# Expert routing with fused VectorE steps, slots rounded to tiles in floating point, and the second layer's input loaded partly in halves

## What is computed

```python
def _moe_ref(x, w_skip, w_gate, w1, w2):
    do_compute = x @ w_skip > 0
    xc = x[do_compute]
    logits = xc @ w_gate
    e_idx = np.argmax(logits, axis=1)
    probs = softmax(logits); gate_w = probs[arange, e_idx]
    y[e_idx == e] = gate_w * (np.maximum(xc @ w1[e], 0.0) @ w2[e])
    out[do_compute] = xc + y            # other rows: out = x

def _moe2_ref(x, w_gate, w_output_gate, w1, w2):
    # the same without the skip and without adding x;
    # y is scaled by gate_w * sigmoid(x @ w_output_gate)[e] as well
```

## Time and profile before

| | |
|---|---|
| median of 3 runs | 690.13 us (688.09 to 690.76) |
| profiled execution | 688.13 us, its span 686.4 us |
| TensorE matmul busy | 658.4 us (96%) |
| TensorE weight load busy | 564.5 us (82%) |
| VectorE busy | 409.9 us (60%) |
| ScalarE busy | 337.0 us (49%) |
| GpSimd busy | 295.2 us (43%) |
| routing of layer 1, first logits step to first w1 matmul | 268.6 to 297.9 us |
| routing of layer 2, load of x issued to first w1 matmul | 434.7 to 469.5 us |

### The profile page before, as it was taken

The page is one execution under the profiler, slowest core; times in us unless marked ns, Lnnn a source line. Parts: engine busy times, 40 slices in busy tenths (PEclk is TensorE's granted clock), DMA queues, the critical chain, the costliest instruction groups (busy, mean ns, idle before and its releaser), DMA issues.

```text
span 686.4 us, 15791 instructions
## 1 busy us (share of the span) xinstructions
PE 658.4 (96%) x5939; PEld 564.5 (82%) x5949; DVE 409.9 (60%) x859; ACT 337.0 (49%) x507; POOL 295.2 (43%) x287
## 2 busy tenths in 40 slices
PE   8989999999999989899999999989999999999995
PEld 5569889888888876479998998547999999999894
DVE  7878888788888857755454635375245254443421
ACT  4568999999999886331334312232213213231200
POOL 4357999989999871021221322002132132122121
PEclk9999999999999999999999999999999999999999
DMA  9301231111220439748489964654545654941000
GB/s 279 94 2 47 55 86 49 47 48 48 60 82 25 143 129 334 280 131 310 160 301 349 349 241 142 233 208 130 192 160 173 248 174 172 372 176 51 19 31 32
DMA packets 45988, 105.77 MB, mean 154 GB/s; under 512 B 5459, under 2 KB 11603, under 8 KB 45936
## 3 DMA queue, kind: packets, MB, share of 16 engines
q1 hardware_dynamic: 38464, 87.65, 36.8%
q0 software_dynamic: 4544, 12.70, 5.8%
q10 hardware_dynamic: 2928, 4.72, 2.0%
HBM read 87.64 MB, written 13.11 MB: 147 GB/s over the span
## 4 chain that ended last, share of the span: by engine, by line
PE 53%; DVE 3%; DMA 2%; issue 1%; ACT 0%; POOL 0%; POOLq 0%; ACTq 0%; DVEq 0%
PE hT_ps_layer L1381 27%; PE y_ps_layer L1394 7%; PE y_ps_layer L1398 7%; PE y_ps_layer L1401 7%; PE x_turn_layer L1368 2%; DMA x<-x_mid 1%; PE hT_ps_layer L1310 1%; PE hT_ps_layer L1308 1%; PE x_turn_layer L1298 1%; DVE row_one_hot_layer L1210 1%; DMA x_tile_layer<-x_src,token_to_read_layer 1%; PE hT_ps_layer L1323 1%; DMA x_mid<-y_out_layer,y_token_layer 0%; PE count_ps_layer L1298 0%; PE rank_ps_layer L1298 0%
## 5 line engine op out<-in xcount | busy, mean ns | idle before, releaser
L1381 PEld LDWEIGHTS hT_ps_layer<-xT_layer,w 128*128 128x128 f32 x1664 | 189.6, 192 | 3.8 <-DVE xT_layer L1243 1.7
L1381 PE MATMUL hT_ps_layer<-xT_layer,w 128*128 128x128 f32 x1664 | 190.2, 275 | 0.8 <-issue 0.8
L438 POOL TENSOR_TENSOR probs_lo<-probs,probs_hi 128x768 f16<-128x768 f32 x89 | 146.1, 1649 | 33.0 <-ACT probs_hi L353 30.4
L1132 ACT ACTIVATE hT_hi_layer<-hT_ps_layer 128x512 fp32r<-128x512 f32 x52 | 31.1, 597 | 239.2 <-PE hT_ps_layer L1381 239.2
L565 DVE TENSOR_REDUCE max_halves<-turn 128x1 f32<-128x384 f32 x180 | 94.7, 553 | 31.8 <-PE turn L729 30.2
L1270 DVE SCALAR_TENSOR_TENSOR hT_lo_layer<-hT_ps_layer,hT_hi_layer 128x512 fp32r<-128x512 f32 x52 | 34.6, 689 | 88.0 <-ACT hT_hi_layer L1132 77.0
L345 ACT ACTIVATE probs<-scores 128x768 f32<-128x768 f32 x96 | 79.9, 832 | 11.3 <-PE scores L753 10.3
L1445 POOL DMA_INDIRECT out_dram<-y_out_layer,y_token_layer x16 | 19.7, 1234 | 147.1 <-DVE y_out_layer L1281 147.1
L353 ACT ACTIVATE probs_hi<-scores 128x768 f16<-128x768 f32 x96 | 80.2, 836 | 1.2 <-PE pv L777 0.9
L1127 ACT ACTIVATE w_hi<-w 128x1024 fp32r<-128x1024 f32 x64 | 62.4, 1047 | 26.6 <-issue 26.6
L1250 DVE TENSOR_TENSOR w_lo<-w,w_hi 128x1024 fp32r<-128x1024 f32 x64 | 74.0, 1219 | 0.0
(11 more groups left out here) (227 smaller groups left out, 1087.5 us busy)
## 6 DMA issues: line engine op xcount, KB each, us to landing
w<-in_moe_w_dram SPq DMA_DIRECT2D x32, 2048.0 KB, 11.2
w<-in_v_dram ACTq DMA_DIRECT2D x4, 768.0 KB, 7.1
qk_raw<-in_q_dram SPq DMA_DIRECT2D x16, 192.0 KB, 3.2
qk_raw<-in_k_dram SPq DMA_DIRECT2D x16, 192.0 KB, 3.5
qB<-qA SPq DMA_DIRECT2D x16, 192.0 KB, 2.7
kB<-kA SPq DMA_DIRECT2D x16, 192.0 KB, 3.1
x_src<-x SPq DMA_DIRECT2D x2, 1536.0 KB, 17.0
x_mid<-x SPq DMA_DIRECT2D x2, 1536.0 KB, 18.3
```

The costliest lines, as they stand in the source:

```text
L438: nc.gpsimd.tensor_tensor(p_lo[slot][:], probs[slot][:], p_hi[slot][:], ALU.subtract).then_inc(p_lo_pool, 1)
L1381: t = nc.tensor.matmul(hp[n][:, i * P:(i + 1) * P], W1[par][:, c, f * P:(f + 1) * P], xT[:, c, :], start=(c == 0), stop=(c == CD - 1))
```

## The change

- The comparison with the maximum is made on `z` (is it 0), in one instruction with the product by the order numbers; the skip is one instruction with the conversion to bf16; the f32 one-hot is gone, the bf16 one is used in its place.
- A slot's tile is found without integers: a large constant, 3 x 128 x 2^22, is added, whose floating-point neighbours are 128 apart, so that the sum is rounded to tiles. The row in the tile comes out negated (`st[:, 2, :]`), and the column numbers run from 0 down to -127, now in bf16.
- The skipped tokens' offset is a ninth column of `slots`, summed with the others.
- The row one-hots are twelve instructions of 128 columns, each with a per-partition scalar, in place of two of 768 columns; TensorE waits for each. They stand ahead of the tile table, which stood ahead of them.
- The sums of the gate (of the exponentials in both layers, of the selected output gate in layer 2) are moved behind the token numbers.
- The first third of x in layer 2 is loaded in two halves of 256 columns on each queue, the second with a semaphore of its own.

```diff
--- before.py
+++ after.py
@@ -18,6 +18,8 @@
 N_EXPERTS = 8
 NO_TILE = 1 << 10
 NO_TOKEN = 1 << 11
+
+TO_TILES = P * 3 << 22
 N_TOKENS = 1536
 
 RING = 4
@@ -956,7 +958,6 @@
 
     TURNS = 4
     NG, GT = NM // 4, 4
-    HM = NM // 2
     wgs = sb("gate_weights_hi_lo", [P, CD, 2 * G], F32R)
     xh = [sb(f"xT_hi{i}", [P, GT * P], F32R) for i in range(TURNS)]
     xl = [sb(f"xT_lo{i}", [P, GT * P], F32R) for i in range(TURNS)]
@@ -964,11 +965,12 @@
     lgs = sb("gate_logits", [P, NM, G], F32)
     eq = sb("gate_best", [P, NM, E], F32)
     eqw = sb("gate_best_first", [P, NM, E], F32)
-    one_hot = sb("expert_one_hot", [P, NM, E], F32)
+    best = sb("expert_best", [P, NM, E], F32)
+
+    slots = sb("expert_slots", [P, NM, E + 1], F32)
     one_hot_b = sb("expert_one_hot_b", [P, NM, E], BF16)
     z = sb("gate_shifted", [P, NM, E], F32)
     st = sb("route_stats", [P, 12, NM], F32)
-    rank_i = sb("rank_in_expert", [P, 3, NM], I32)
     count = sb("expert_count", [P, 4, E], F32)
     over = sb("over", [P, E, thr.shape[1]], F32)
     before = sb("tiles_before", [P, E, E], F32)
@@ -1079,10 +1081,14 @@
         for par in range(2):
             expert(E // 2 - 1, par)
 
+    X_PARTS = (2, 1, 1)
+
     def x_group(dma, b, g):
 
         src = x_copy.rearrange("(b p t) d -> b p t d", b=Xt.shape[2], p=P)[b][:, 2 * g:2 * g + 2, :]
-        dma.dma_start(Xt[:, 2 * g:2 * g + 2, b, :], src).then_inc(x_loaded[g], 16)
+        for i in range(X_PARTS[g]):
+            d = slice(i * DM // X_PARTS[g], (i + 1) * DM // X_PARTS[g])
+            dma.dma_start(Xt[:, 2 * g:2 * g + 2, b, d], src[:, :, d]).then_inc(x_loaded[g if i == 0 else NG], 16)
 
     with nc.Block() as blk:
         @blk.sync
@@ -1156,27 +1162,21 @@
             gate = lgs[:, :, gate_at:gate_at + E]
             link(nc.vector.tensor_reduce(st[:, 0, :], gate, AX.X, ALU.max))
             nc.vector.tensor_tensor(z[:], gate, bc(st[:, 0, :]), ALU.subtract).then_inc(shifted, 1)
-            link(nc.vector.tensor_tensor(one_hot[:], gate, bc(st[:, 0, :]), ALU.is_equal))
-
-            link(nc.vector.tensor_tensor(eqw[:], one_hot[:], tie[:, 0:E].unsqueeze(1).to_broadcast([P, NM, E]), ALU.mult))
+            dve.wait_ge(shifted, 1)
+            link(nc.vector.scalar_tensor_tensor(out=eqw[:], in0=z[:], scalar=0.0, in1=tie[:, 0:E].unsqueeze(1).to_broadcast([P, NM, E]),
+                                                op0=ALU.is_equal, op1=ALU.mult))
             link(nc.vector.tensor_reduce(st[:, 1, :], eqw[:], AX.X, ALU.max))
-            link(nc.vector.tensor_tensor(one_hot[:], eqw[:], bc(st[:, 1, :]), ALU.is_equal))
             if first:
-                link(nc.vector.tensor_scalar(st[:, 2, :], lgs[:, :, 0:1].rearrange("p m o -> p (m o)"), 0.0, None, ALU.is_gt))
-                link(nc.vector.tensor_tensor(one_hot[:], one_hot[:], bc(st[:, 2, :]), ALU.mult))
-            nc.vector.tensor_copy(one_hot_b[:], one_hot[:]).then_inc(mask_done, 1)
+                link(nc.vector.tensor_tensor(best[:], eqw[:], bc(st[:, 1, :]), ALU.is_equal))
+                nc.vector.scalar_tensor_tensor(out=one_hot_b[:], in0=lgs[:, :, 0:1].to_broadcast([P, NM, E]), scalar=0.0, in1=best[:],
+                                               op0=ALU.is_gt, op1=ALU.mult).then_inc(mask_done, 1)
+            else:
+                nc.vector.tensor_tensor(one_hot_b[:], eqw[:], bc(st[:, 1, :]), ALU.is_equal).then_inc(mask_done, 1)
 
 
             if first:
 
-                link(nc.vector.tensor_scalar(st[:, 11, :], st[:, 2, :], -float(P * NO_TILE), float(P * NO_TILE), ALU.mult, ALU.add))
-            else:
-                link(nc.vector.tensor_tensor(eqw[:], one_hot[:], lgs[:, :, E:2 * E], ALU.mult))
-                link(nc.vector.tensor_reduce(st[:, 5, :], eqw[:], AX.X, ALU.add))
-                dve.sem_inc(sel_done, 1)
-            dve.wait_ge(exp_done, 1)
-            link(nc.vector.tensor_reduce(st[:, 3, :], eq[:], AX.X, ALU.add))
-            link(nc.vector.tensor_scalar_add(st[:, 4, :], st[:, 3, :], 1e-9))
+                link(nc.vector.tensor_scalar(slots[:, :, E:E + 1], lgs[:, :, 0:1], 0.0, float(P * NO_TILE), ALU.is_le, ALU.mult))
 
 
             K = thr.shape[1]
@@ -1192,29 +1192,36 @@
             dve.wait_ge(ranked, 1)
             link(nc.vector.scalar_tensor_tensor(out=eqw[:], in0=count[:, 3, :].unsqueeze(1).to_broadcast([P, NM, E]), scalar=float(P),
                                                 in1=rank_ps, op0=ALU.mult, op1=ALU.add))
-            link(nc.vector.tensor_tensor(eqw[:], eqw[:], one_hot[:], ALU.mult))
-            link(nc.vector.tensor_reduce(st[:, 9, :], eqw[:], AX.X, ALU.add))
-            if first:
-                link(nc.vector.tensor_tensor(st[:, 9, :], st[:, 9, :], st[:, 11, :], ALU.add))
-            link(nc.vector.tensor_copy(rank_i[:, 0, :], st[:, 9, :]))
-            link(nc.vector.tensor_scalar(rank_i[:, 2, :], rank_i[:, 0, :], 7, None, ALU.logical_shift_right))
-            nc.vector.tensor_scalar(rank_i[:, 1, :], rank_i[:, 0, :], P - 1, None, ALU.bitwise_and).then_inc(row_known, 1)
+            some = slice(0, E + 1 if first else E)
+            link(nc.vector.tensor_tensor(slots[:, :, 0:E], eqw[:], one_hot_b[:], ALU.mult))
+            link(nc.vector.tensor_reduce(st[:, 9, :], slots[:, :, some], AX.X, ALU.add))
+
+            link(nc.vector.tensor_scalar(st[:, 11, :], st[:, 9, :], 0.5 - P / 2, float(TO_TILES), ALU.add, ALU.add))
+            nc.vector.scalar_tensor_tensor(out=st[:, 2, :], in0=st[:, 11, :], scalar=float(TO_TILES), in1=st[:, 9, :],
+                                           op0=ALU.subtract, op1=ALU.subtract).then_inc(row_known, 1)
             wide = lambda a: a.unsqueeze(2).to_broadcast([P, NM, NT_COLS])
-            link(nc.vector.tensor_tensor(tile_hot[:], wide(rank_i[:, 2, :]), tile_no[:].unsqueeze(1).to_broadcast([P, NM, NT_COLS]), ALU.is_equal))
+            link(nc.vector.tensor_tensor(tile_hot[:], wide(st[:, 11, :]), tile_no[:].unsqueeze(1).to_broadcast([P, NM, NT_COLS]), ALU.is_equal))
             nc.vector.tensor_tensor(tile_tok[:], tile_hot[:], wide(tok_no[:]), ALU.mult).then_inc(toks_hot, 1)
+
+            dve.wait_ge(row_known, 1)
+            for m in range(NM):
+                nc.vector.tensor_scalar(row_hot[:, m, :], cols[:], st[:, 2, m:m + 1], None, ALU.is_equal).then_inc(rows_hot, 1)
             link(nc.vector.tensor_scalar_add(count[:, 2, :], count[:, 1, :], 1.0))
             link(nc.vector.tensor_copy(table[:], count[:, 2:4, :]))
             dve.sem_inc(table_done, 1)
-            dve.wait_ge(row_known, 1)
-            for m in range(0, NM, HM):
-                nc.vector.tensor_tensor(row_hot[:, m:m + HM, :], rank_i[:, 1, m:m + HM].unsqueeze(2).to_broadcast([P, HM, P]),
-                                        cols[:].unsqueeze(1).to_broadcast([P, HM, P]), ALU.is_equal).then_inc(rows_hot, 1)
 
 
             dve.wait_ge(toks_turned, 1)
             nc.vector.tensor_scalar(read_tok[:], tok_ps, float(NO_TOKEN), float(n_tok - 1), ALU.add, ALU.min).then_inc(to_read, 1)
             nc.vector.tensor_scalar(send_tok[:], tok_ps, float(NO_TOKEN), None, ALU.add).then_inc(to_send, 1)
 
+            if not first:
+                link(nc.vector.tensor_tensor(eqw[:], one_hot_b[:], lgs[:, :, E:2 * E], ALU.mult))
+                link(nc.vector.tensor_reduce(st[:, 5, :], eqw[:], AX.X, ALU.add))
+                dve.sem_inc(sel_done, 1)
+            dve.wait_ge(exp_done, 1)
+            link(nc.vector.tensor_reduce(st[:, 3, :], eq[:], AX.X, ALU.add))
+            link(nc.vector.tensor_scalar_add(st[:, 4, :], st[:, 3, :], 1e-9))
             if first:
                 link(nc.vector.reciprocal(st[:, 8, :], st[:, 4, :]))
             else:
@@ -1290,8 +1297,8 @@
         def _(pe):
             def route_turn(k):
                 g, c = divmod(k, CD)
-                if not first and c == 0:
-                    pe.wait_ge(x_loaded[g], 32)
+                if not first and c * X_PARTS[g] % CD == 0:
+                    pe.wait_ge(x_loaded[g if c == 0 else NG], 32)
                 if k >= TURNS:
                     pe.wait_ge(r_lo, k - TURNS + 1)
                 for i in range(GT):
@@ -1348,8 +1355,7 @@
 
             pe.wait_ge(toks_hot, 1)
             for m in range(NM):
-                if m % HM == 0:
-                    pe.wait_ge(rows_hot, m // HM + 1)
+                pe.wait_ge(rows_hot, m + 1)
                 t = nc.tensor.matmul(tok_ps, row_hot[:, m, :], tile_tok[:, m, :], start=(m == 0), stop=(m == NM - 1))
             t.then_inc(toks_turned, 1)
             warm(8)
@@ -1480,10 +1486,10 @@
         tie_b = sb("tie_b", [P, C], BF16)
         thr = sb("thresholds", [P, K_THR], F32)
         below = sb("experts_before", [P, E, E], F32)
-        cols = sb("column_number", [P, P], F32)
+        cols = sb("column_number_below_zero", [P, P], BF16)
         tri = sb("partitions_above", [P, P], BF16)
         ones_b = sb("ones_b", [P, P], BF16)
-        tile_no = sb("tile_number", [P, NT_COLS], F32)
```

(7 more changed lines are left out.)

## The result

Over 22 executions each, the kernel after took 691.97 us (median) and the one before 690.47: a ratio of 1.0033 with an interval of 1.0019 to 1.0047. The prediction had 689.0 against 690.13, a ratio of 0.998. So it was wrong: a gain of 1.1 us was forecast, and a loss was measured, of 1.5 us by the medians and of 2.3 by the ratio. The miss is 2.6 to 3.4 us. The profiled execution took 692.57 us (before: 688.13), with a span of 690.8 and a granted clock of 0.989 (before: 0.998).

What follows compares the result with a forecast made beforehand. The prediction took TensorE's gapless expert tiles as untouched, so only the two routing stages between them could change. Layer 1 -1.18, layer 2 -0.20, halves +0.30 gave -1.1 us: 689.0 against a median of 690.13, range 686.3 to 691.0.

Steps and rivals of the forecast that it cites:

- a wait or an allocation moves work elsewhere: Rival: the change is not what it seems, or over 3.4 us comes from the tile loops; either way, 5%.
- A, from the logits to the counts: Routing, z to the first step on the counts: shorter by 0.70 us in layer 1, 0.96 in layer 2.
- B, from the ranks to the one-hots: Routing, line 1193 to the first row one-hot: shorter by 0.93 us in layer 1, 0.72 in layer 2.
- C and D, the one-hots and what follows: Twelve row one-hots take 2.24 us, not 1.84, losing 0.40 a layer; from there to the token numbers costs 0.02.
- rivals at 0.106 and at 0.27 apart: Row one-hots: at 0.106 us each, 687.2 us in all (20%); at 0.27 each, 691.1 us (10%).
- The token numbers: VectorE's token numbers in routing start 1.21 us earlier in layer 1 and 1.26 in layer 2.
- E, the moved sums: Gate sums behind token numbers: 0.49 us in layer 1, nearly covered; 1.06 in layer 2, all paid, first tile gains 0.20.
- F, the halves: Layer 2's load of x, first third in halves: second group lands later, costing 0.3 us, bounds 0 and 0.5.
- the first group's arrival is worth nothing: Layer 2's load of x: TensorE waits again for the second group, so only that one's arrival counts.
- gate path isn't what layer 2 waits for: Rival, layer 2 routing: fillers shrink or the gather rules, so the moved 1.06 us is hidden; 688.0 us, 10%.
- halves gain 0.3: Rival, layer 2's load of x: first steps start earlier, second group no later; 0.3 us gained, 688.4 us, 12%.
- slow one-hots: Rival: row one-hots run at the two-tensor rate plus the scalar, 3.3 us a layer; 691.1 us, 10%.

Runs made afterwards that it cites:

- after + 32 bytes: Kernel after with 32 unused bytes a partition ahead of hT_hi in layer 2, no instruction changed: 690.14 us, 0.9989 of the kernel before.
- after + fillers: Kernel after with 14 blank matmuls instead of 8 behind the token numbers, layer 2 only: 690.2 us, 0.9998 of the kernel before.
- before + gap: Kernel before with 2 blank matmuls instead of 8 behind the token numbers in layer 2: 692.14 us, 1.0034 of the kernel before.
- 32 bytes ahead of x: Kernel after with 32 unused bytes a partition ahead of x, moving everything behind it: 691.76 us in one execution.

## Why the prediction was wrong

- **What bounds the kernel.** The tile loops were taken as a row of TensorE work that the change can't touch. It touched them by where its tensors lie: +1.5 us in layer 2 (after + 32 bytes takes it back), about -0.4 in layer 1. The rival "a wait or an allocation moves work elsewhere" named it at 5%, without a price.
- **A, from the logits to the counts.** Right: -0.63 (forecast -0.70) and -0.97 (-0.96). The 0.07 in layer 1 is a slip of the sum: the mask at 283.41 instead of 284.05 is 0.64, and the counting behind it didn't change.
- **B, from the ranks to the one-hots.** Right: -0.92 (-0.93) and -0.71 (-0.72). Prices of dependent steps, read from rows 4 and 5, carried over to the new ones here within 0.01 us in all.
- **C and D, the one-hots and what follows.** Right in kind; the term was mis-sized. The twelve start 0.163 us apart and are 248 ns long, 2.04 us where 2.24 were forecast, and the stretch to the token numbers grew by 0.24 and 0.25 instead of 0.42. The rivals at 0.106 and at 0.27 apart both fall. By the Trainium skill's rate for bf16 ("VectorE: DVE Perf Modes", section "The perf-mode tier table") the prediction's estimate was 0.17, and that was the nearer one.
- **The token numbers.** 1.31 and 1.44 us earlier, forecast 1.21 and 1.26.
- **E, the moved sums.** Layer 1 right: -1.34 in all against -1.18. In layer 2 the delay was right: token numbers to first transposes grew by 1.19 us (after + fillers, 5.83 against 4.64), forecast 1.06. (Some 0.4 of it came back between the transposes and the first w1 matmul, which is 7.34 us behind the token numbers instead of 6.55.) The step that failed stands one sentence on: "All of the 1.06 is paid: the token numbers gain 1.26, the first tile gains 0.20." It took an idle TensorE for a mere delay. Its wait ahead of the gate matmuls became 2.59 us long, and behind it fillers and transposes ran at 1.2 GHz: 1.2 + 0.5 = 1.7 us more, shown by before + gap and by after + fillers. At the full clock the first tile does gain, 0.64 us; with the clock lost it is 1.03 later. The prediction had the idle time in its rows and let the clock be, because the profiled execution had 1.00 in both routing stages.
- **F, the halves.** Right in sign, short in size: 0.5 to 0.65 us of load where 0.30 was forecast, and 0.99 in the profiled pair. The prediction priced the packets and kept the further issue for its upper bound of 0.5; the second group was in fact issued 0.54 us later, and its load took 0.11 longer, where 0.3 was put on the packets. The step that failed besides is "the first group's arrival is worth nothing": it is worth less than nothing, since an early start only makes the wait behind it longer, and behind that wait the clock fell in four profiles of eight, 1.6 us each time.
- **The median and the profile.** The 2.0 us between them were carried along as they were. They are the clock that most executions lose, mostly in attention: 0.994 against 0.998 is 2.8 us of 690. The prediction could have asked what this one execution lacked.
- **The sum.** Of the 2.6 to 3.4 us missed, the clock at layer 2's gate is 1.7, in full, since a fall there cost the kernel before nothing; the tiles are 1.5 - 0.4 = 1.1; the halves' load 0.2 to 0.35 beyond the forecast, and the clock behind them 4/8 x 1.6 = 0.8; the routing steps were better than thought by 0.16 and 0.44. That makes 3.2 to 3.4 us, and the interval of the ratio is 1.0 us either way. The shares of executions that lose the clock come from few profiles each and are the weak part of this sum: in attention, without fillers there, it fell in 6 of 9 profiles built on the kernel after and in 2 of 4 built on the one before.

The rival that the gate path isn't what layer 2 waits for fell: the chain still goes over the gate parts. The rival that the halves gain 0.3 fell as well. That of slow one-hots had a time near the measured one (691.1), by luck: its mechanism didn't happen.

## What to carry to other kernels

Where a step is moved, check what the engine behind it does while it waits: a longer idle TensorE doesn't only cost its length, it can cost the clock of what follows, and a few blank matmuls over the wait give that back. Don't read a clock of 1.00 in one execution as a property of the kernel; set the profiled execution's time against the median and ask what the difference is made of. Any edit that adds or resizes a buffer can move hot operands against one another, so compare the period of an untouched loop before and after, and if it differs try a pad before blaming an instruction.

## What the runs showed of the hardware

- The granted clock fell to 0.50 (1.2 GHz) for 3.4 us (6.8 in before + gap) at idle times of TensorE of 2.5 to 2.6 us ahead of the gate matmuls, in seven profiles of seven, and in four of eight behind 1.7 to 3.2 us at the load of x in halves. With 1.3 us or less ahead of the gate and added fillers it held in six of six. No length of the wait alone separates the cases: it held behind 2.23 us in after + fillers and fell behind 2.15 in the kernel with 32 bytes ahead of x.
- In attention the clock fell in 8 of 13 profiles without fillers there and in 1 of 5 with them (mean clock 0.997 against 0.994), and cost up to 2.5 us. The waits ahead don't tell which: 1.59 and 1.11 us in the kernel before, where it held, 1.59 and 0.82 in the kernel after, where it fell.
- In layer 2, weights and streamed operand that begin in different halves of 64 bytes cost 4 ns for each 512-column matmul with a weight load, 0.10 us or 0.8% of a tile. The Trainium skill says in "TensorE: Matmul & The Clock Gate", section "Step-by-step: what each phase is for", that the engine reads weights and stream over two ports of their own and that loading the next weights takes nothing from the running matmul. Here the same instructions took 13.08 and 13.18 us a tile by the two operands' places alone. If that is these two reads meeting, the measurement decides against the sentence; that it is, is argued, not shown.
- A VectorE comparison of 128 bf16 columns with a per-partition scalar takes 248 ns and starts 0.163 us behind the one ahead, against 286 ns for line 520's f32.
